# Who empties a gram first, and where a solve stands among the products: a reordering in a fused attention and expert kernel

## The reference

```python
k_n = k / (norm(k) + 1e-6)                       # B=4, H=8, S=768, D=48
for t in range(S):                                # a delta rule
    y[t] = q[t] @ state
    state += beta[t] * outer(k_n[t], v[t] - k_n[t] @ state)
x = y as [3072, 384]
h = ((x @ w1) * (x @ w2)) @ w3                    # d_ff = 1024
x = h @ w_out
logits = x @ phi                                  # 32 slots
d = softmax of logits over the tokens; slot_in = d.T @ x
slot_out = relu(slot_in @ e1[e]) @ e2[e]          # 8 experts of 4 slots
out = softmax of logits over the slots @ slot_out
```

## Time and profile before

| | |
|---|---|
| median of 3 runs | 501.59 us (499.52 to 505.74) |
| the profiled execution | 501.76 us |
| its span, first to last instruction | 500.0 us |
| granted TensorE clock, mean over the span | 0.976 |
| PE busy | 452.2 us, 90% |
| DVE, ScalarE, GpSimd busy | 49%, 46%, 38% |

### The profile page before, as it was taken

The page is one execution under the profiler, slowest core; times in us unless marked ns, Lnnn a source line. Parts: engine busy times, 40 slices in busy tenths (PEclk is TensorE's granted clock), DMA queues, the critical chain, the costliest instruction groups (busy, mean ns, idle before and its releaser), DMA issues.

```text
span 500.0 us, 21358 instructions
## 1 busy us (share of the span) xinstructions
PE 452.2 (90%) x9729; PEld 325.1 (65%) x9729; DVE 247.3 (49%) x499; ACT 227.7 (46%) x408; POOL 188.7 (38%) x329
## 2 busy tenths in 40 slices
PE   4665899999999999999999999999979999999982
PEld 3333467767767777777677776767767777754442
DVE  3899596357443665536373462843441332144123
ACT  1234465636545645455455553555534553424112
POOL 1001499811688215884038860188800000000000
PEclk9995999999999999999999999999999999999997
DMA  7999305400024400154000640000170085699949
GB/s 196 385 232 342 83 5 126 119 16 3 3 63 87 110 5 3 28 106 128 4 3 3 128 130 4 5 3 3 44 297 1 4 335 173 208 413 430 421 177 372
DMA packets 21002, 64.96 MB, mean 130 GB/s; under 512 B 2352, under 2 KB 3760, under 8 KB 20016
## 3 DMA queue, kind: packets, MB, share of 16 engines
q1 hardware_dynamic: 20208, 62.71, 38.7%
q10 hardware_dynamic: 704, 0.89, 0.7%
HBM read 58.87 MB, written 4.72 MB: 127 GB/s over the span
## 4 chain that ended last, share of the span: by engine, by line
PE 71%; POOL 6%; DMA 6%; DVE 5%; issue 4%; SPq 4%; ACT 1%; DVEq 0%; POOLq 0%
PE pA L1221 17%; PE pB L1221 17%; PE pKY L1123 4%; PE pD L1157 4%; PE pKY L1138 4%; DMA step_slab<-e_dram 3%; PE pKY L1172 3%; POOL prep_slab L486 3%; POOL prod_p L485 3%; DMA arena<-kq_dram 3%; PE pT L1237 3%; PE pG L1237 2%; PE pD L1245 2%; SPq L358 2%; PE pT L1107 2%
## 5 line engine op out<-in xcount | busy, mean ns | idle before, releaser
L485 POOL TENSOR_TENSOR prod_p<-prep_slab 128x30 f32<-128x30 f32 (+9 forms) x150 | 75.9, 506 | 47.5 <-DVE prep_slab L820 36.6
L753 DVE TENSOR_TENSOR arena<-a_sb,pB 128x512 f32<-128x512 f32 x41 | 28.2, 687 | 127.5 <-PE pB L1221 127.0
L486 POOL TENSOR_TENSOR prep_slab<-prep_slab,prod_p 128x30 f32<-128x30 f32 (+9 forms) x150 | 82.1, 548 | 11.7
L524 ACT ACTIVATE step_slab<-pKY 32x384 f32<-32x384 f32 x92 | 44.4, 483 | 33.8 <-PE pKY L1172 32.1
L1221 PE MATMUL pB<-whi,xhi 128*128 128x512 f32 x135 | 55.9, 414 | 0.0
L1221 PE MATMUL pB<-whi,xlo 128*128 128x512 f32 x135 | 53.5, 396 | 0.0
L1221 PE MATMUL pB<-wlo,xhi 128*128 128x512 f32 x135 | 52.7, 391 | 0.0
L1221 PE MATMUL pA<-whi,xhi 128*128 128x512 f32 x135 | 52.1, 441 | 0.0
L1221 PE MATMUL pA<-wlo,xhi 128*128 128x512 f32 x135 | 47.1, 401 | 0.0
L1221 PE MATMUL pA<-whi,xlo 128*128 128x512 f32 x135 | 46.6, 399 | 0.1
L466 POOL TENSOR_TENSOR arena<-arena,nrm 128x1152 f32<-128x1152 f32 (+1 forms) x11 | 21.1, 1914 | 47.0 <-DVE prep_slab L842 46.3
(11 more groups left out here) (284 smaller groups left out, 899.3 us busy)
## 6 DMA issues: line engine op xcount, KB each, us to landing
arena<-e_dram SPq DMA_DIRECT2D x7, 1536.0 KB, 14.5
arena<-kq_dram SPq DMA_DIRECT2D x44, 192.0 KB, 6.0
late_w<-e_dram SPq DMA_DIRECT2D x4, 1536.0 KB, 10.2
arena<-kv_dram SPq DMA_DIRECT2D x6, 768.0 KB, 5.4
arena<-kv_dram SPq DMA_DIRECT2D x24, 192.0 KB, 5.7
arena<-w3t_dram SPq DMA_DIRECT2D x2, 2048.0 KB, 20.0
arena<-w_dram SPq DMA_DIRECT2D x1, 4096.0 KB, 13.8
out_dram<-late_w SPq DMA_DIRECT2D x6, 576.0 KB, 5.5
```

Source lines behind the costliest of these rows:

```text
L485: link(nc.gpsimd.tensor_tensor(pv, a, x, ALU.mult))
L486: link(nc.gpsimd.tensor_tensor(dst, dst, pv, ALU.add))
L524: nc.scalar.activation(xs[quad(b), :], pKY[quad(quarter(g, b) ^ 1), bank(g, b), 0:DM], ACT.Copy).then_inc(y_done, 1)
L753: nc.vector.tensor_tensor(ab_tile(s, p)[:, half * HF:(half + 1) * HF], a_sb[:], up_bank(t, half, 1), ALU.mult).then_inc(ab_done, 1)
```

## The change

Five edits, all of order and of waits; one operation is replaced.

1. ScalarE's `gram_out` waits for the products alone, and DVE's `mask_pt` waits for ScalarE's copy of the same bank (`gs_done`). What reuses a bank now waits for the mask: `grams` for the second pair, `ab_turn` and, in steps 8, 12 and 16, `x_turn`.
2. Mask 3 moves behind `set_up` in DVE's queue, in steps 8, 12 and 16.
3. GpSimd's affine select waits for all five links of `set_up` instead of two.
4. The diagonal in `scale` is written by a `tensor_tensor` (max of beta with itself) instead of a copy.
5. `solve_rows` stands two products further back in steps 8, 12 and 16, and five further back in step 20.

```diff
-                pool.wait_ge(prep_link, prep_base(n) + 2)
+                pool.wait_ge(prep_link, prep_base(n) + ROOT_SPLIT)
...
-                act.wait_ge(*((gram_done, STEPS + 2 * (i // 2 + 1)) if n == 1 else (pt_mask, n * STEPS + i + 1)))
+                act.wait_ge(gram_done, n * STEPS + 2 * (i // 2 + 1))
...
-                dve.wait_ge(gram_done, n * STEPS + 2 * (i // 2 + 1))
+                dve.wait_ge(gs_done, n * STEPS + i + 1)
...
-                nc.vector.tensor_copy(xs_.rearrange("p a b -> p (a b)")[:, 0:C * C:C + 1], sys_s[:, 4]).then_inc(x_link, 1)
+                nc.vector.tensor_tensor(xs_.rearrange("p a b -> p (a b)")[:, 0:C * C:C + 1], sys_s[:, 4], sys_s[:, 4],
+                                        ALU.max).then_inc(x_link, 1)
...
                     if n != 1:
                         mask_at(2)
-                        mask_at(3)
...
                     if s == 0 and prep:
                         set_up(n + 1, q, k)
+                        if n > 1:
+                            mask_at(3)
...
                     if pair > 0:
-                        pe.wait_ge(gs_done, n * STEPS + 2)
+                        pe.wait_ge(pt_mask, n * STEPS + 2)
...
                 pe.wait_ge(gs_done, grams_before)
+                if grams_before > 2 * STEPS:
+                    pe.wait_ge(pt_mask, grams_before)
...
-                        up(t, 0, 1, None, 0, 2)
+                        up(t, 0, 1, None, 0, 4)
                         solve_rows(g, p, s, n)
-                        up(t, 0, 1, None, 2)
+                        up(t, 0, 1, None, 4)
...
+                        ahead = 5 if s == 0 and is_last(n) else 0
+                        if ahead:
+                            up(t, 0, 1, sums, 0, ahead)
                         solve_rows(g, p, s, n)
-                        up(t, 0, 1, sums)
+                        up(t, 0, 1, sums, ahead)
...
+                    if s == 0 and prep:
+
+                        pe.wait_ge(pt_mask, made - 1)
                     x_turn(g)
```

## The result

The changed kernel takes 499.39 us (median of 20 runs, 497.61 to 500.75) where the kernel before, on the same chip, takes 502.25 (497.87 to 506.15): ratio 0.9947, 95% interval 0.9928 to 0.9967. That is 2.7 us less by the ratio, within 2%, and inside my range. But I had forecast no gain, and the sign was the other one. A few runs of some kernels lie more than 1.5% above the fastest of the same kernel; the ratios here leave them out, the medians and ranges of runs do not.

The account below looks back on a forecast made before the run. PE was taken to bound the kernel, busy 452.2 of 500.0 us. Step 4's +0.3 and zeros elsewhere gave 502.1 us on the profiled execution, 501.9 as the forecast median; range 499.0 to 505.0.

Parts of the forecast that it names:

- its end stays: Step 20, state_step: the 2.56 us gap ends when w3's load lands; PE would reach it 0.5 us earlier and wait longer.
- the gap goes: Rival, chance 0.06: the 42 waits shift where PE runs out of instructions, gap and low clock vanish, 497.1 us.
- Mostly hidden: Skill's rule on the cost of going between instruction blocks; by it step 20's 0.52 us would be kept.
- no engine released those: PE's "issue" waits ahead of state_step, 6.7 us in 6 places: released by no engine, untouched by the edits.
- Step 4: Masks behind ScalarE's copies make R 0.8 us later; an "issue" wait may cover part: +0.3 us, bounds 0.1 to 0.8.
- Steps 8, 12, 16: Masks there stand behind R and hold back only the second pair's grams, much later: price 0.
- the solve two products later: Steps 8, 12, 16: five products, 1.26 us, still cover Z's copy of 0.80 us: price 0.
- Mask 3, select, Newton: Steps 8, 12, 16: DVE gains at most 0.17 us, held by ScalarE's a_sb; price 0, bounds 0 and -0.5.
- The diagonal: scale, step 19: the max waits for GpSimd's scaling as the copy did, 2.0 us; price 0 on PE.
- Step 20, five products ahead: Solve's 0.52 us wait is filled, but PE then waits as much longer in the gap: 0, bounds -0.52 and 0.
- The waits: 42 satisfied mask waits in PE's queue cost nothing: 0; upper end 0.09 us each, 3.8 us.
- 'issue' waits as a whole change by over 2 us: Sign that would show the forecast wrong: PE's instruction waits in total change by more than 2 us.

Follow-up runs that it names:

- the copy: The kernel before, run and profiled a second time without any change of order (FILLERS 46 + 1): 502.54 us, ratio 1.002.
- e1: The kernel before with only five products put ahead of the solve in step 20: 500.58 us, ratio 0.9936.
- e8: The changed kernel with FILLERS 47 -> 31, 64 instructions fewer at the very start: 505.33 us, ratio 1.0089 to the kernel before.
- e7: The kernel before with the load of w3 issued one step later, behind step 20's last product: 500.64 us, ratio 0.9951.
- e3: The changed kernel with no products put ahead of the solve in step 20: 500.16 us, ratio 0.9979 to the kernel before.
- e5: The changed kernel with right sides R ahead of masks 0 and 1 in step 4: 496.66 us, ratio 0.9853 to the kernel before.
- e6: The kernel before with only the change's 42 already fulfilled mask waits added to PE's queue: 498.76 us, ratio 0.9901.
- e9: The changed kernel with R first in step 4, but diagonal copied, mask 3 and select's release as before: 496.48 us, ratio 0.9914 to the kernel before.
- e12: The kernel before with 29 fulfilled waits (15 instructions in the trace) at one place in step 19: 499.82 us, ratio 0.9961.
- e11: The kernel before with FILLERS 54, 28 instructions more at the very start: 502.37 us, ratio 0.9993.
- e2: The kernel before with FILLERS 47 -> 63, 64 instructions more at the very start: 501.55 us, ratio 1.0016.

## Why the prediction was wrong

**The step that failed: step 20's gap taken as fixed ("its end stays"), and with it the 0 for step 20 and the 0 for the waits.** I saw the gap end 0.02 us after w3 landed and took the load's end for what releases PE. Where the gap stands, the two do fall together: its end is 0.01 to 0.13 us behind w3's landing in before, the copy, e1 and e8. But in e7 it is 0.5 us behind, and there too PE went on 2.50 us after its block began to move. So it is the block that PE waits for. In the changed kernel, and in e3, e5, e6 and e9 to e12, the block came while w3 was loading, so there was no gap to end. Whether it does changes with the number of instructions ahead: before has the gap, e6 (29 more by then, no other edit) and e12 (15 more) do not. The two terms at 0 measured -4.87 us in the profile (step 20) and -5.0 us by the ratio (the waits alone, e6).

**The rival I gave 0.06 ("the gap goes").** I named it, with the right cause (waits are instructions) and nearly the right size (4.8 us; step 20 lost 4.87), and argued it away: 30 instructions at 34 a microsecond move PE by one microsecond, not ten. The arithmetic holds and the conclusion does not. The block was not late in proportion: from before to e12 a quarter of a microsecond at PE went with four at the block. I had no reason to think the gap was far from such an edge, and should have given that rival as much as the forecast.

**"Mostly hidden".** The Trainium skill (Runtime: NRT & Kernel Launch, Instruction fetch mechanics) says so of the step from one block to the next. The trace of before agrees for 70 of 77 block ends, at which it has no "issue" wait of PE over 0.15 us. It does not at the start (5.88 us), nor beside the 4 MB load: there it cost PE 1.64 to 3.49 us in five traces, and in four of them the clock behind it.

**"Issue", 6.7 us in 6 places, "no engine released those".** For four of the six this was wrong. They stand ahead of the first of the 64 products, in steps 5, 9, 13 and 17, 0.85 to 1.18 us each in before and 0.71 to 1.16 in the changed kernel. `state_step` waits there for ScalarE's exponential of the logits (`et_done`, L1148 and L563). These rows of before, timeline of ScalarE and PE, are of step 5:

```profile
128.93 0.20 ACT L562 ACTIVATION_READ_ACCUMULATOR ET<-pD,run 128x1 f32 x1
129.24 0.93 PE L1157 MATMUL pD<-step_slab,arena 32*48 32x48 f32 x64 [1.18 <-issue]
```

The first weight load began at 129.21, 0.07 us after ScalarE's read ended, and it is 0.07 us in all four steps of all the traces. So only the gap and 0.34 us in step 4 were instructions that had not come.

**Step 4: forecast +0.3, bounds 0.1 to 0.8.** That R comes 0.8 us later was right. That the "issue" wait behind would cover most of it was not: it grew to 1.01 us. In the two profiles the step is 1.37 us longer, above my upper bound: 0.82 us ahead of the solve, and 0.55 at the two block ends of this step. Over all kernels the order of the kernel before gives a step 4 of 20.9 us (mean of 8, 19.56 to 21.67), the changed order 21.5 (mean of 3), rows first 19.75 (mean of 3). By these means the change cost about +0.6, inside the bounds, and less than the scatter of the kernels among each other. What I missed is that DVE's order there was already wrong before: R ahead of the masks is worth about 1.1 us against the old order, 1.8 against the new.

**Steps 8, 12, 16 and the solve two products later: 0.** Right: 19.00, 19.79 and 20.61 us against 18.98, 20.31 and 20.51, and the copy's step 12 moved by -0.35 us and e6's by -0.78. The 0.5 us in step 12 are the block-end wait that the changed kernel does not have there.

**Mask 3, select, Newton: 0.** Right, in its rows (L792 0.18 us, L753 held by a_sb) and nearly so in the steps (e9).

**The diagonal: 2.0 us, price 0.** Right: 2.02 us, all six of its instructions as before within 0.03 us. These are the groups of L842 and L792 in the changed kernel (shortest, median, longest in ns, first and last start):

```profile
L842 DVE TENSOR_TENSOR prep_slab<-sys_s x6: 221/2021/2027, 46.9 to 364.3; 128x32 f32<-128x32 f32 x6
```
```profile
L792 DVE TENSOR_SCALAR sys_s<-sys_s x6: 181/182/182, 17.6 to 318.6; 128x32 f32<-128x32 f32 x6
```

The rule of the Trainium skill (SBUF — State Buffer, Who interferes with whom) holds for this operation with two inputs of SBUF: 0.22 us with GpSimd at rest and 2.02 beside its scaling. One reading of mine was off: L839 takes 1.22 us beside GpSimd's scaling and 1.22 where GpSimd rests, so of that pair only GpSimd lost time.

**Step 20, five products ahead: 0 of -0.52.** Right as long as the gap stands (e1), wrong without it: 14.98 us in the changed kernel, 15.58 in e3. Since the gap went, 0.6 us were kept in the profile.

**The waits: 0.** As waits, right in e6. In a row, 29 of them took 1.4 us (e12), 0.05 us a wait or 0.1 us an instruction, the order of my upper end of 0.09. Spread over the steps they are hidden. As instructions they were the largest term of all, and its sign was a gain.

**The sum.** In the profiles: step 20 -4.9, step 4 +1.4, step 3 +0.9, step 23 +0.7, steps 12 and 22 -1.0, start +1.6: -1.3 with the small ones, the 1.3 us by which the spans differ (500.0 and 498.7). The start and part of the rest moved as much in the copy. From the ratios: the waits alone -5.0 us (e6; 3.3 to 6.6), the whole change -2.7 (1.7 to 3.6). Whether the rest of the change gives anything back is not shown: the two intervals meet, and the medians are 0.6 us apart. My sign "'issue' waits as a whole change by over 2 us" did not come, the shorter gap did.

**What stays open.** Why a block begins to move either about 4 us or less, or over 7 us, after PE has passed the boundary: no run measured what the instruction queue waits for. How much of the time is the gap's: step 20 is 4.1 to 4.9 us shorter in the traces of six kernels without it, and by the ratios their times differ from before by -5.0 (e6), -2.7 (the change), -1.9 (e12), -1.1 (e3), -0.4 (e11) and +0.8 us (e2). That they keep or lose it in every execution was not traced. Why e2 and e11 lost the gap and no time: the longer start (64.00, 63.45 against 61.38 and 62.98) and step 23 are in their profiles, but the start scatters by 1.6 us without an edit, and I had one profile of each. And how far e5 and e9 owe their time to step 4 alone: the profile says 1.8 us against the changed kernel, the medians 2.7 and 2.9, and their ratios (0.9853 and 0.9914 against 0.9947) 4.7 and 1.6.

## What to carry to other kernels

An "issue" wait in the middle of a row of equal products was PE waiting for instructions in every case here; ahead of the first of a row it could be a semaphore (steps 5, 9, 13, 17), so look at the waits in the source. Count PE's queue up to it and run a copy with some instructions more at a place just ahead, before pricing any edit: an edit of no cost that changes the count can be worth more than all that it was made for, and the gain may go with the next edit. Moving the load moved the gap and shortened it (e7); moving the count took it away. And where one queue serves a copy, a mask and the operand of the next product, the operand goes first: step 4 was 1.8 us shorter for it on the mean, and e5, the change with this order, took 496.66 us, 0.9853 of the kernel before.

## What the runs showed of the hardware

- Beside a 4 MB load a block of PE's instructions moved 2.8 to 4.0 us after PE had passed the beginning of the block before it, or 7.1 to 7.3 us after; the nearest two traces of either kind are a quarter of a microsecond apart at PE (4.24 and 3.99 us after the load's issue). Where PE had run out, it went on 2.50 to 2.64 us after the block began to move.
- PE standing for 2.56 us was followed by a granted clock of 0.53 for 3.6 us. After 1.64 us (e7), and without the gap, it stayed at 1.00.
- 29 fulfilled waits in a row, 15 instructions in the trace, kept PE for 1.4 us; 42 spread over the steps from 4 on for no time that shows.
- A `tensor_tensor` of 128x32 with both inputs in SBUF took 2.02 us beside GpSimd's scaling and 0.22 with GpSimd at rest; a `tensor_scalar` of the same size (L792) took 1.22 us beside GpSimd's affine select and 0.18 without it.
- The same program's start took 61.38 and 62.98 us in two profiled executions, more than most edits here are worth.
